# Local attention in tiles of 24 queries and 32 keys in an attention and two-layer expert kernel on one core

## What is computed

```python
q_d, k_d, v_d = means over 4 neighbouring tokens            # 144 tokens
out_up = repeat(softmax(q_d @ k_d.T / 8) @ v_d, 4)
mask = abs(pos[:, None] - pos[None, :]) < 4                 # a band of 7 keys
out_local = softmax(where(mask, q @ k.T / 8, -1e9)) @ v
x = (out_up + out_local)  ->  2304 tokens x 512
h = x @ w_in;  x = (h * clip(h + 3, 0, 6) / 6) @ w_out      # 512 -> 2048 -> 512
out = max(x @ w1, x @ w2, x @ w3) @ w_out2                  # 512 -> 768 -> 512
```

## Time and profile before

| | us |
|---|---|
| median of 3 runs (773.39 to 774.57) | 773.63 |
| profiled execution, its own time | 774.09 |
| its span, first to last instruction | 772.3 |

### The profile page before, as it was taken

One profiled execution on the slowest core, in us unless ns is written; L12 is line 12 of the kernel. 1 busy time (PEld: TensorE's weight loads), 2 busy tenths in 40 slices (PEclk: granted clock), 3 DMA queues, 4 the chain that ended last, 5 costly groups with the idle time before them and its releaser, 6 DMA issues.

```text
span 772.3 us, 13368 instructions
## 1 busy us (share of the span) xinstructions
PE 756.3 (98%) x5254; PEld 670.6 (87%) x5254; DVE 435.1 (56%) x822; ACT 285.7 (37%) x623; POOL 221.0 (29%) x280
## 2 busy tenths in 40 slices
PE   7889999999999999999999999999999999999998
PEld 5667777878888788778999999999989999899996
DVE  5866676367556646653556756266771656535650
ACT  4845544343343334334444435222241221412211
POOL 7864866321122022201247650022200111011110
PEclk9999999999999999999999999999999999999999
DMA  9994633223302331301436886787014750137202
GB/s 182 190 235 101 157 64 65 48 70 64 64 18 47 84 83 21 61 18 56 177 115 260 306 330 215 255 344 257 30 41 130 279 192 1 56 123 279 103 2 81
DMA packets 123851, 100.48 MB, mean 130 GB/s; under 512 B 89996, under 2 KB 108428, under 8 KB 123788
## 3 DMA queue, kind: packets, MB, share of 16 engines
q1 hardware_dynamic: 121108, 98.75, 42.1%
q10 hardware_dynamic: 2680, 0.89, 0.6%
HBM read 73.66 MB, written 25.95 MB: 129 GB/s over the span
## 4 chain that ended last, share of the span: by engine, by line
PE 89%; DVE 4%; POOL 3%; ACT 1%; DMA 1%; issue 1%; SPq 1%; DVEq 0%; POOLq 0%
PE bank L885 28%; PE bank L886 27%; PE bank L887 27%; PE bank L1025 1%; PE bank L1002 1%; PE bank L991 1%; DMA k_nat_c<-in_k_dram 1%; PE bank L947 1%; PE bank L964 1%; PE bank L977 1%; POOL w L798 1%; POOL dp_a L790 1%; SPq L519 0%; ACT dp_a L1251 0%; ACT rg L1319 0%
## 5 line engine op out<-in xcount | busy, mean ns | idle before, releaser
L885 PE MATMUL bank<-xo,wt 128*128 128x384 f32 x378 | 126.3, 334 | 0.0
L887 PE MATMUL bank<-xo,wt 128*128 128x384 f32 x378 | 126.3, 334 | 0.0
L886 PE MATMUL bank<-xo,wt 128*128 128x384 f32 x378 | 126.3, 334 | 0.0
L1688 DVE SCALAR_TENSOR_TENSOR rg<-rg,bank 128x512 f32<-128x512 f32 (+1 forms) x80 | 50.5, 632 | 127.1 <-ACT rg L1319 126.8
L885 PE MATMUL bank<-xs,w 128*128 128x512 f32 (+1 forms) x320 | 120.9, 378 | 0.9 <-DVE xs L1656 0.9
L885 PE MATMUL bank<-gs,w 128*128 128x512 f32 (+1 forms) x320 | 120.4, 376 | 0.6 <-DVE y L1702 0.5
L887 PE MATMUL bank<-xs,w 128*128 128x512 f32 (+1 forms) x320 | 118.0, 369 | 0.0
L886 PE MATMUL bank<-xs,w 128*128 128x512 f32 (+1 forms) x320 | 117.9, 368 | 0.0
L886 PE MATMUL bank<-gs,w 128*128 128x512 f32 (+1 forms) x320 | 117.7, 368 | 0.0
L887 PE MATMUL bank<-gs,w 128*128 128x512 f32 (+1 forms) x320 | 117.6, 368 | 0.0
L1319 ACT ACTIVATE rg<-bank,half 128x512 f32<-128x512 f32 (+1 forms) x80 | 51.5, 644 | 150.1 <-PE bank L887 150.1
(11 more groups left out here) (252 smaller groups left out, 1137.2 us busy)
## 6 DMA issues: line engine op xcount, KB each, us to landing
wt<-t_scratch SPq DMA_DIRECT2D x19, 1792.0 KB, 7.6
t_scratch<-ph SPq DMA_DIRECT2D x9, 896.0 KB, 3.6
t_scratch<-pl SPq DMA_DIRECT2D x9, 896.0 KB, 5.7
b_raw<-in_moe_w_dram SPq DMA_DIRECT2D x9, 512.0 KB, 4.0
xr<-x_scratch SPq DMA_DIRECT2D x3, 1536.0 KB, 10.0
out_dram<-o_sb SPq DMA_DIRECT2D x18, 256.0 KB, 2.0
w_raw<-in_moe_w_in_dram SPq DMA_DIRECT2D x16, 256.0 KB, 3.9
w_raw<-in_moe_w_out_dram SPq DMA_DIRECT2D x16, 256.0 KB, 4.9
```

The costliest lines, as they stand in the source:

```text
L885: mm(dst, w[0], m[0], start=start, stop=False, skip_group_check=True)
L886: mm(dst, w[0], m[1], start=False, stop=False, skip_group_check=True)
L887: return mm(dst, w[1], m[0], start=False, stop=stop, skip_group_check=True)
L1688: vec.scalar_tensor_tensor(out=gated(s), in0=gated(s), scalar=1.0, in1=hidden_bank(s)[:, 0:n], op0=ALU.min, op1=ALU.mult).then_inc(s_g, 1)
```

## The change

The local tiles become 24 queries by 32 keys. 24 tiles are spread over the four quarters of the partitions, six to a quarter, so that a tile's scores are a block of 32 by 32. scores_local has 48 matmuls of 64 dimensions, 32 queries and 32 keys. DVE turns the blocks in one instruction (turn_local on DVE), the PE transposes and their copies on ACT are gone, and values_local has 48 matmuls of 32 keys and 24 queries. It runs in two parts, quarters 0 and 1 and then 2 and 3, which write the same banks. The second waits for the first. put_x has two instructions. The local tensors have 2 x 6 x 32 = 384 columns. There is one mask for both heads, made once by POOL and turned to bf16 by DVE. The bands of values are eight transfers a pair.

The orders are also new: keep_warm reads a zeroed tile of its own and no longer waits for POOL, scores_down(0) is ahead of turn_q(2) on PE, k(2) is loaded by ACT's queue and v4(0) by SP's, sum_v stands behind the norms on POOL, low_w1 releases hidden after its first half and stands behind attend(2s + 1), and in step 1 attend(2) is behind add_out(1).

```diff
-    KW = 64
-    QW = 58
-    NT = 10
-    TPH = NT // 2
+    KW = 32
+    QW = 24
+    NT = S // QW
+    QUARTERS = P // KW
+    TPH = NT // QUARTERS
...
-    mask = work("mask", [P, 2, TPH, KW])
+    mask = work("mask", [P, TPH, KW])
...
+                    for i in range(QUARTERS):
+                        rows = to.vb[i * KW:(i + 1) * KW, h]
+                        lo, hi = 0, TPH
...
+                        sp.dma_start(rows[:, lo:hi, :], band(TPH * i + lo, hi - lo)).then_inc(to.s_vb, 16)
...
             load_q(2)
-            load_k(2)
+            load_v4(0)
+            load_k(3)
+            load_v4(1)
             load_vb(0)
-            load_v4(1)
-            load_vb(1)
             load_v4(2)
             load_q(3)
-            load_k(3)
+            load_w1(0)
+            load_vb(1)
+            load_v4(3)
             load_vb(2)
-            load_w1(0)
-            load_v4(3)
+            load_w1(1)
             load_vb(3)
-            load_w1(1)
             load_w1(2)
...
-                if pieces[-1] == 3:
-                    mine.then_inc(s_w1, 1)
+                    if i == 1:
+
+                        mine.then_inc(s_w1, 1)
+                    if i == 3:
+                        mine.then_inc(s_w1o, 1)
...
-            sum_v(0)
             norm_local(0)
             norm_down(0)
+            sum_v(0)
+            norm_local(1)
             sum_v(1)
             sum_v(2)
-            norm_local(1)
             norm_down(1)
             norm_local(2)
+            norm_down(2)
+            low_w1(0, (0, 1))
+            low_w1(0, (2, 3))
             sum_v(3)
-            norm_down(2)
-            low_w1(0)
+            norm_down(3)
             norm_local(3)
-            norm_down(3)
-            low_w1(1)
-            low_w1(2)
+            low_w1(1, (0, 1))
+            low_w1(2, (0, 1))
+            low_w1(1, (2, 3))
+            low_w1(2, (2, 3))
             for s in range(STEPS):
                 attend(2 * s)
+                attend(2 * s + 1)
                 if s + 3 < F1:
                     low_w1(s + 3)
-                attend(2 * s + 1)
...
+                for i in range(TPH):
+                    for quarter in range(QUARTERS):
                         for h, dst in enumerate((t.ba, t.bb)):
-                            a = QW * tile_of(h, x, i)
+                            a = QW * (TPH * quarter + i)
                             rows = slice(h * D, (h + 1) * D)
-                            mine = mm(dst[x * KW:(x + 1) * KW, i * KW:(i + 1) * KW], t.qT[rows, a:a + KW],
-                                      t.kT[rows, a:a + KW], start=n >= PAIRS, stop=True, skip_group_check=True)
+                            mine = mm(dst[quarter * KW:(quarter + 1) * KW, i * KW:(i + 1) * KW],
+                                      t.qT[rows, a:a + KW], t.kT[rows, a:a + KW], start=n >= PAIRS, stop=True,
+                                      skip_group_check=True)
...
+            def values_local(n, part):
...
+                if part == 0:
+
+                    pe.wait_ge(s_cd, n + 1)
+                    pe.wait_ge(s_lt, n + 1)
+                    pe.wait_ge(to.s_vb, band_of(n))
...
+                else:
+
+                    pe.wait_ge(s_pvq, n + 1)
+                for i in range(TPH):
+                    for h in range(2):
+                        for quarter, dst in ((2 * part, t.ba), (2 * part + 1, t.bb)):
+                            rows = slice(quarter * KW, (quarter + 1) * KW)
+                            at = SD * part + QW * i
+                            mine = mm(dst[h * D:(h + 1) * D, at:at + QW], to.vb[rows, h, i, :],
+                                      t.lT[rows, h, i, 0:QW], start=True, stop=True, skip_group_check=True)
+                mine.then_inc((s_pvq, s_pv)[part], 1)
+
+            def values(n):
+                values_local(n, 0)
                 if narrow(n):
...
+                    values_local(n, 1)
+                    values_down(n)
+                else:
+                    values_down(n)
+                    values_local(n, 1)
...
+            pe.wait_ge(s_still, 1)
+            keep_warm(20)
             pe.wait_ge(s_ident, 1)
-            keep_warm(30)
             turn_q(0)
             turn_k(0)
             turn_q(1)
             scores_local(0)
             turn_k(1)
+            scores_down(0)
             turn_q(2)
             scores_local(1)
             turn_k(2)
-            scores_down(0)
             scores_local(2)
-            keep_warm(14)
-            turn_local(0)
+            keep_warm(8)
             turn_down(0)
+            keep_warm(8)
             scores_down(1)
-            values_down(0)
-            values_local(0)
+            values(0)
             scores_down(2)
-            keep_warm(8)
             turn_q(3)
-            turn_local(1)
             turn_k(3)
             turn_down(1)
+            keep_warm(4)
             scores_local(3)
-            values_down(1)
-            keep_warm(4)
-            turn_local(2)
-            values_local(1)
+            values(1)
+            turn_down(2)
+            keep_warm(8)
             scores_down(3)
-            turn_down(2)
-            keep_warm(12)
-            hidden(0, range(0, 2))
-            turn_local(3)
-            values_down(2)
+            values(2)
+            hidden(0, range(0, 1))
             turn_down(3)
-            values_local(2)
-            values_down(3)
-            values_local(3)
+            hidden(0, range(1, 2))
+            values(3)
             hidden(1, range(0, 2))
             hidden(0, range(2, 3))
             hidden(1, range(2, 3))
+            hidden(2, range(0, 1))
             hidden(0, range(3, 4))
+            hidden(2, range(1, 3))
             hidden(1, range(3, 4))
-            hidden(2)
+            hidden(2, range(3, 4))
...
+            copy_q(0)
...
             copy_q(1)
             copy_k(1)
+            exp_local(0)
             copy_q(2)
-            exp_local(0)
+            exp_down(0)
             copy_k(2)
...
+            def turn_local(n):
+                t = tiles(n)
+
+                dve.wait_ge(s_lnorm, n + 1)
+                vec.transpose(t.lT[:].rearrange("p h t w -> p (h t w)"),
+                              t.lp[:].rearrange("p h t w -> p (h t w)")).then_inc(s_lt, 1)
...
-            pool_qk(0)
+            pool_q(0)
+            pool_k(0)
+            pool_q(1)
             max_masked(0)
             sub_masked(0)
-            pool_qk(1)
+            pool_k(1)
             max_down(0)
             inverse_local(0)
             max_masked(1)
             inverse_down(0)
             sub_masked(1)
-            pool_qk(2)
+            turn_local(0)
+            pool_q(2)
+            inverse_local(1)
             max_masked(2)
             max_down(1)
```

More of the change, by code:

```diff
@@ L89, in attention_moe_kernel @@
     HALO = FACTOR - 1
-    KW = 64
-    QW = 58
-    NT = 10
-    TPH = NT // 2
-    COLS = [min(QW, S - QW * i) for i in range(NT)]
-    PADW = QW * (NT - 1) + KW
-    LOWER = [6, 4]
-    NV = max(LOWER)
-    def tile_of(h, x, t):
-        upper = (t + h) % 2
-        return upper * LOWER[h] + 2 * (t // 2) + x
-    def at_tile(h, i):
-        x, t = next((x, t) for x in range(2) for t in range(TPH) if tile_of(h, x, t) == i)
-        block, rows = divmod(TPH * h + t, 2)
-        assert rows == (i >= LOWER[h])
-        return block, rows, x
+    KW = 32
[3 more added lines that the diff above has]
+    TPH = NT // QUARTERS
+    PADW = S + KW - QW
     J = 6
@@ L294, in working @@
                 dinv=work(f"dinv{tag}", [DT, 4]),
-                ba=bank[a], bb=bank[b], bc=bank[a if c is None else c], l4=l4, d0=d0, d1=d1, pd=pd)
+                ba=bank[a], bb=bank[b], bc=bank[a if c is None else c], d0=d0, d1=d1, pd=pd)
         land_a = landing("_a")
@@ L434, in attention_moe_kernel @@
         s_pvd = sem("s_pvd")
+        s_pvq = sem("s_pvq")
         s_pv = sem("s_pv")
@@ L887, in three @@
                 return mm(dst, w[1], m[0], start=False, stop=stop, skip_group_check=True)
-            idle = ident[:].bitcast(mybir.dt.bfloat16)
+            idle = still[:]
             def keep_warm(count, dst=STEP0):
@@ L1176, in _ @@
                 add_out(s)
+                if s == 1:
+                    attend(2 * s)
                 attend(2 * s + 1)
```

224 lines of the change are left out of this document (86 added, 138 removed).

## The result

The changed kernel takes 792.18 us (median of 4 runs, 790.26 to 799.31) against 773.59: 1.0257 times as long, with a 95% interval of 1.0218 to 1.0295. The forecast was 769.6, faster. The profiled execution took 791.32 us for a span of 789.2.

The account below looks back on a forecast made before the run. TensorE, busy 98% of the span, was taken to bound the kernel. 774.09 - 3.4 (lead-in) - 2.0 (loop stalls) + 1.3 (pair blocks) = 770.0, median 0.46 below: 769.6 us; forecast 767.5 to 771.5, range 765.5 to 778.

Parts of the forecast that it names:

- 12 x 0.027 + 0.20 = 0.52 us: Local scores of a looped pair: twelve rounds on eight tiles, 0.52 us in place of 0.75, -0.2 us a pair.
- paid by the record: Slower rival, chance 0.16: small matmuls cost per record, 0.95 to 1.25 us more a pair for scores, 781 to 785 us.
- Turn -0.54, values +0.85: Per looped pair: five local transposes go, -0.54 us; values become two parts of 0.85 us, 1.70 in place of 0.85.
- The floor of 25 ns: Skill's objection, set aside: matmul starts never under about 25 ns apart, so 96 records take 2.4 us, scores add 20 us.
- Together I take -2.0 us: TensorE's loop stalls behind VectorE and POOL shrink or go through the new order: -2.0 us, ends 0 and -2.5.
- if the next w1 were late in the new order: Loop, low_w1 behind the norms: the case where the stall gain is zero; set against hidden having two steps of time.
- it has the whole slot: Loop: VectorE's turn of 384 columns is covered between norm_local and values; without cover about 0.5 us a pair.
- Lead-in, -3.4: Stretch before the loop: new order gains 3.4 us, taken from a hand walk's -4.2; ends -6 and +1.
- The walk: Hand trace of the lead-in's new order with today's durations: hidden(3) at 56.6 us in place of 60.78, -4.2 us.
- if a granted clock of 0.5 stands over 41 to 48 us: Sign that the forecast is wrong: TensorE at half clock over the big matmuls that end the lead-in.
- 1.7 us in a rival: No-change rival, chance 0.2: lead-in gives nothing back, a 3.4 us low-clock stretch over big matmuls costing 1.7 us; 773 us.
- v_band_c: Sign that the forecast is wrong: TensorE stands for this lead-in band load, expected near 33.5 us where values(2) wants it.

Follow-up runs that it names:

- b_pool_order: The kernel before with one loop move: GpSimd makes low_w1 after both attend slots of a step; 777.69 us, ratio 1.0050.
- b_step1: The kernel before with one loop edit: in step 1 the first attend slot comes behind add_out on TensorE (ScalarE, VectorE likewise); 776.55 us, ratio 1.0043.
- b_records_96: The kernel before with 28 small idle matmuls ahead of scores of pairs 0 to 3 and values of 0 and 1, making 96 records a block; 775.43 us.
- a_half_records: The changed kernel with half of the local score and value matmuls of pairs 0 to 3 left out; 788.55 us, ratio 1.0184 to the kernel before.
- old_lead: The changed kernel's tiles and loop with the lead-in order of before on all engines and the load queue; 791.40 us, ratio 1.0227 to the kernel before.
- scores_twice: The changed kernel with each of the 96 local score matmuls of the twelve looped pairs issued twice; 816.32 us, ratio 1.0536 to the kernel before.
- scores_half: The changed kernel with a second set of looped pairs' local score matmuls that passes 16 columns in place of 32; 815.12 us (one run).

## Why the prediction was wrong

It said 774.09 - 3.4 - 2.0 + 1.3. Measured against the profiled spans it is + 8.4 (lead-in), + 8.5 (rest). Point by point:

- **Scores, "12 x 0.027 + 0.20 = 0.52 us": wrong.** Mis-sized: the block is 1.04 where I forecast about 0.6 in the same measure, +0.21 us a pair in place of -0.2. I let the weight columns alone set the round, however many tiles share it, and took the lower end, "because the round has the same length with two tiles busy and with four". With eight tiles and half the weight columns a round of eight records takes 67 ns (8 x 8.3), where 27 were forecast and four tiles with 64 weight columns take 58. The rival "paid by the record" was nearer in kind and had too high a price (0.0135 us a record was its lower end, 0.0083 is measured), so it too missed the loop's share, 5.5 us.
- **Turn -0.54, values +0.85: right.** Measured -0.54 and +0.79. The round of 0.054 us for 64 weight columns, which the values rest on, is 0.058 in the trace.
- **The floor of 25 ns.** A set of 96 records is 48 matmuls in 0.80 us: 8.3 ns a record, 16.7 ns a matmul. The Trainium skill (TensorE: Matmul & The Clock Gate, section "Wait — 56ns, not 53.3ns?") says that start to start never drops below about 25 ns, however few the columns. Its warning pointed the right way and I set it aside; its figure doesn't hold for tiles that run side by side.
- **"Together I take -2.0 us" for the stalls: wrong.** The waits that I counted are gone or smaller, four new ones are there, and the sum fell by 0.4 us only (3.3 to 2.9). I priced what each edit removes and asked too little who comes next. For low_w1 I named the right question ("if the next w1 were late in the new order") and answered it from its two steps of time; b_pool_order shows that it is late, 3.2 us of it. For step 1, b_step1 shows the wait of 1.45 coming back as 3.26.
- **What I had not thought of: VectorE held by GpSimd.** 5.31 us for 0.68, and through the turn's place in VectorE's queue 1.50 us of TensorE and 3.2 us of clock. I had costed VectorE's turn at nothing because "it has the whole slot"; it hasn't when the instruction ahead of it takes 5 us. The trace agrees with the Trainium skill (SBUF — State Buffer, section "SBUF: two separate sides") that a VectorE instruction with two inputs in SBUF is held off by one of GpSimd that reads there. The Trainium skill has the hold last for that one instruction; here it went on through several back to back.
- **Lead-in, -3.4: wrong, and the largest step, 11.8 us.** The walk was right to within a microsecond at its first point (scores_down(0) at 13.01, 12.25 forecast) and 4 us late at the third (scores_down(1) 24.04 for 19.9), with one wait (0.78 us), one stop inside a run of records (1.74) and 3.4 us at the lower clock in between. From 31 us on TensorE waited for nobody up to the cut. The prediction's test, "if a granted clock of 0.5 stands over 41 to 48 us", came true, over 30.15 to 50.63. Its length and price were the error: I put it at nothing in the sum and allowed 1.7 us in a rival, for one stretch of 3.4 us over big matmuls; it was 20.5 us long and cost some 8.6 us.
- **v_band_c** did not make TensorE wait. It landed at 33.0.

Shown by runs: what a small record costs in either form; that the lead-in's loss is there with the tiles and the old order; that doubling records makes stops without a releaser; that VectorE's long subtraction comes from GpSimd's order; that the loop edits each lose by themselves; that the lower clock in the loop costs 3.5 us. Worked out and not shown: that the lower clock is nearly the whole 8.4 us ahead of the cut. Waits and full-clock work come out equal in the two traces, but the price of a low microsecond there lies between 0.26 and 0.44 us by the way it is taken, and nothing lets me set the clock. Why the clock was low is open as well: small records do not bring it about by themselves (b_records_96 has none of it), nor do the stops without a releaser alone (a_half_records has none of those in its lead-in and 37.5 us at the lower clock). Open too: why runs of 96 records did so little in b_records_96 and so much in old_lead. The second also has the values of pairs 2 and 3, VectorE's turns in its queue and eight band loads for four; these I didn't take apart. And it is open why the same stop at 80 us was followed by 6.8, 3.4 or no us at the lower clock in kernels with the same loop on TensorE.

## What to carry to other kernels

Count records before cutting a matmul into smaller tiles: side by side they cost 15 ns each here with 64 weight columns and 8 ns with 32, whatever number of columns passes, so halving the tile while the records go from 40 to 96 is a loss. Before moving an instruction past another, find out who stands behind it in its new place; all three order edits that promised a gain in a timeline of before (-1.6, -1.45, -1.5 to -3) cost 1.5 to 4 us when made alone. And cut both traces at one common point and compare the two parts: here half of the loss was on either side, one half mostly clock, the other mostly records.

## What the runs showed that I had not expected

- **TensorE seems to run out of instructions.** In nine of the kernels stops without a releaser lie inside or right behind long runs of small records, and in the kernel before there is none. TensorE's instruction queue (q8 on the page: 41 packets before, 55 changed, 64 in scores_twice) brings 16,384 bytes at a time, which is some 128 records (0.67 MB for 5254 of them, an estimate from the page). All 29 such stops of over 0.4 us, in all nine kernels, ended 2.2 to 3.1 us after the start of such a packet (for instance 117.52 and 119.81, 146.34 and 148.90, 18.77 and 21.49). The stop near 80 us, which is VectorE's doing, ended 9 us or more behind the last packet in every kernel that has it. At 8.3 ns a record a packet's worth of small ones is used up in 1.1 us, faster than that. That the missing instructions are the cause is inferred from this, and from the same four stops in scores_twice and scores_half, which have as many records with half the columns passing in a set.
- **A stop of 1.5 to 2.6 us is often followed by the lower clock, and not always.** It was in the changed kernel at 80.45 and, from within the wait, at 31.05; it was not in old_lead, scores_twice and scores_half behind 1.53 to 1.54 us at the place of the first, nor in the kernel before behind 1.45 us at 57.26. In the changed kernel it came back at 50.63, after hidden had begun at 46.77, with TensorE 95% busy through the 20 us before; at 16.49 it had come back in the middle of the small scores of pair 1. So I can't say what a block of small tiles does to it.
- **One VectorE instruction stood eight times its length** (5.31 us for 0.68), beside a run of eight GpSimd subtractions that started 0.12 us earlier, and the profile shows it as busy, not as waiting.
